# Transposing the activation tiles on the Vector engine instead of TensorE, with transfers that put the blocks in place

## What is computed

```
for t in range(S):                       # per batch and head
    m_new = max(f[t] + m, i[t])
    C = exp(f[t] + m - m_new) * C + exp(i[t] - m_new) * outer(v[t], k[t])
    n = exp(f[t] + m - m_new) * n + exp(i[t] - m_new) * k[t]
    y[t] = sigmoid(o[t]) * (C @ q[t]) / max(|n . q[t]|, 1)
x1 = y as 3072 x 320
x2 = square(relu(x1 @ w_in)) @ w_out
out = elu(x2 @ w2_in) @ w2_out
```

## Time and profile before

| | |
|---|---|
| median of three executions | 845.18 us (845.06 to 847.85) |
| the profiled execution, its own time | 846.34 us |
| its span from first to last instruction | 844.2 us |
| mean granted TensorE clock | 0.982 |
| busy: TensorE, Vector, ScalarE, GpSimd | 834.5, 467.6, 491.7, 264.3 us |

### The profile page before, as it was taken

One profiled execution on the slowest core, in us unless ns is written; L12 is line 12 of the kernel. 1 busy time (PEld: TensorE's weight loads), 2 busy tenths in 40 slices (PEclk: granted clock), 3 DMA queues, 4 the chain that ended last, 5 costly groups with the idle time before them and its releaser, 6 DMA issues.

```text
span 844.2 us, 14970 instructions
## 1 busy us (share of the span) xinstructions
PE 834.5 (99%) x5568; PEld 822.1 (97%) x5568; DVE 467.6 (55%) x823; ACT 491.7 (58%) x1088; POOL 264.3 (31%) x291
## 2 busy tenths in 40 slices
PE   8999999999999999999999999999999999999998
PEld 7899999999999999999999999999999999999998
DVE  5898776665675766656636644444434344444442
ACT  5698676767766767677648754444444444444443
POOL 2654221322222222211102353333334333333332
PEclk7599999999999999999999999999999999999999
DMA  8785444453643443436132300000000000000000
GB/s 252 243 233 147 116 115 108 113 141 90 165 123 105 111 117 108 112 102 159 31 103 76 97 1 2 24 1 24 1 24 1 24 1 24 1 23 3 1 24 24
DMA packets 28257, 66.93 MB, mean 79 GB/s; under 512 B 9401, under 2 KB 15385, under 8 KB 25625
## 3 DMA queue, kind: packets, MB, share of 16 engines
q1 hardware_dynamic: 27608, 64.54, 26.9%
q10 hardware_dynamic: 576, 1.44, 0.5%
HBM read 60.87 MB, written 4.03 MB: 77 GB/s over the span
## 4 chain that ended last, share of the span: by engine, by line
PE 89%; DVE 6%; ACT 2%; issue 1%; DMA 1%; POOL 0%; ACTq 0%; DVEq 0%
PE hps L933 40%; PE acc L947 38%; PE att L858 4%; PE att L823 2%; PE att L849 2%; PE att L863 1%; PE att L838 1%; DVE gate L618 1%; DVE win L690 1%; ACT wts L469 1%; DVE glo L773 1%; DMA wts<-m_rows 1%; PE att L864 1%; DVE win L688 1%; DVE x L673 0%
## 5 line engine op out<-in xcount | busy, mean ns | idle before, releaser
L933 PE MATMUL hps<-xth,win 128*128 128x384 f32 x1280 | 350.6, 339 | 1.0 <-DVE hact L798 1.0
L947 PE MATMUL acc<-wout,ghi 128*128 128x320 f32 x1536 | 347.4, 313 | 0.0
L933 PE MATMUL hps<-xtl,win 128*128 128x384 f32 x768 | 259.9, 338 | 0.0
L947 PEld LDWEIGHTS acc<-wout,ghi 128*128 128x128 f32 x1536 | 257.8, 188 | 0.3 <-POOL glo L431 0.3
L947 PE MATMUL acc<-wout,glo 128*128 128x320 f32 x768 | 237.3, 309 | 0.0
L933 PEld LDWEIGHTS hps<-xth,win 128*128 128x128 f32 x1280 | 229.8, 189 | 1.4 <-issue 1.2
L431 POOL TENSOR_TENSOR glo<-hact,ghi 128x384 fp32r<-128x384 f32 x128 | 130.1, 1016 | 218.6 <-ACT ghi L593 218.5
L773 DVE TENSOR_TENSOR glo<-hact,ghi 128x384 fp32r<-128x384 f32 x128 | 80.1, 626 | 146.5 <-ACT hact L550 145.0
L933 PEld LDWEIGHTS hps<-xtl,win 128*128 128x128 f32 x768 | 145.0, 189 | 0.0
L588 ACT ACTIVATE hact<-hact 128x384 f32<-128x384 f32 x128 | 67.3, 526 | 131.9 <-DVE hact L795 131.9
L947 PEld LDWEIGHTS acc<-wout,glo 128*128 128x128 f32 x768 | 144.1, 188 | 0.0
(11 more groups left out here) (136 smaller groups left out, 665.9 us busy)
## 6 DMA issues: line engine op xcount, KB each, us to landing
raw<-in_qk SPq DMA_DIRECT2D x20, 960.0 KB, 7.2
wts<-m_rows SPq DMA_DIRECT2D x24, 512.0 KB, 8.5
kvo<-in_kvo SPq DMA_DIRECT2D x21, 484.0 KB, 7.9
x<-in_w_all SPq DMA_DIRECT2D x12, 352.0 KB, 7.5
wts<-in_w_all SPq DMA_DIRECT2D x12, 352.0 KB, 2.9
q_of_three<-in_q_trios SPq DMA_DIRECT2D x20, 180.0 KB, 2.6
out_x<-hsum SPq DMA_DIRECT2D x16, 160.0 KB, 1.9
x<-in_w_all ACTq DMA_DIRECT2D x4, 352.0 KB, 6.7
```

Of the source, the lines that this page charges most:

```text
L933: last = nc.tensor.matmul(hps[t % 2][:, 0:NT], win[:, j, w, :], x[:, kk, :], start=(i == 0), stop=(i == len(parts) - 1))
L947: last = nc.tensor.matmul(acc[u][:, 0:DM], g[t % GR][:, cols], wout[:, j, w, :], start=(j == 0 and i == 0), stop=(j == NF - 1 and i == 2))
```

## The change

- **Layer 1, tiles 6 to 23.** At delay 4 the Vector engine transposes the tile by quadrants of 32 partitions: 16 instructions of 32 x 96 elements (`turned`), each of which puts its 32 x 32 blocks on the partitions where they belong, into a new buffer `x1_turned`. `x_hi` and `x_lo` at delay 5 then read that buffer and not PSUM. TensorE's transposes stay for tiles 0 to 5 alone.
- **Layer 2, all 24 tiles.** The Vector engine transposes every 32 x 32 block where it stands (`x2_turned`: two instructions, 320 and 64 elements). Then 16 transfers from SBUF to SBUF on SyncE's queue, 32 partitions and three runs of 128 B each, bring the blocks to their partitions in `x1` (`move_x2`). `x2_hi` and `x2_lo` read from there. The turning stands four steps ahead of its use (`X2_AHEAD`), and `X2_STEPS` is now 5, 9 and 13. A tile is turned only once the transfers of the tile before have landed, as there is one buffer.
- **SyncE's queue** issues the moves between the weight loads of block 7 and the output stores.
- **The last weight slice's** low part on the Vector engine goes from step 0 of block 8 to step 3.
- GpSimd's `copy_rest` goes away, and `m0` lies in another buffer.

```diff
-X2_STEPS = (7, 9, 11)
+X2_STEPS = (5, 9, 13)
+X2_AHEAD = 4
+TURNED = 4
+def turned_at(t):
+    g = tile_at(t, TURNED)
+    return g if g is not None and g >= 2 * T else None
...
+            def move_x2(i):
+                sp.wait_ge(s["x2_turned"], i + 1)
+                wait(sp, "xt_ready", TILES + i - 1)
+                whole = x1[i % 2][:].rearrange("f (k t) -> f k t", t=P)
+                for a in range(4):
+                    for q in range(4):
+                        rows = slice(a * 32, (a + 1) * 32)
+                        sp.dma_start(whole[q * 32:(q + 1) * 32, :, rows], x2_blocks[rows, q::4, :]).then_inc(s["x2_moved"], 16)
...
             wait(sp, "intra_ps", TILES)
-            for n in range(NF, 2 * NF):
-                load_w(sp, n)
+            for n in range(NF, NF + SPARE - 2):
+                load_w(sp, n)
+            for j in range(NF):
+                if j + X2_AHEAD in X2_STEPS:
+                    move_x2(X2_STEPS.index(j + X2_AHEAD))
+                if SPARE - 2 <= j + SPARE - 2 < NF:
+                    load_w(sp, NF + j + SPARE - 2)
+            for block in range(BLOCKS, 2 * BLOCKS):
+                for w in range(T):
+                    if block < 2 * BLOCKS - 1:
+                        move_x2(T * (block + 1 - BLOCKS) + w)
+                    if w == 0 and block > BLOCKS:
+                        for u in range(T):
+                            store(T * (block - 1 - BLOCKS) + u)
...
+            def x2_hi(i, par, u):
+                act.wait_ge(s["x2_moved"], 256 * (i + 1))
+                nc.scalar.activation(xth[par][:, :, u * P:(u + 1) * P], x1[i % 2][:].rearrange("d (k t) -> d k t", t=P), ACT.Copy)\
+                    .then_inc(s["xth_ready"], 1)
...
+            def turned(src, dst, a):
+                rows = src[a * 32:(a + 1) * 32, :].rearrange("t (b f) -> t b f", f=32)
+                blocks = dst.rearrange("f (k t) -> f k t", t=P)[:, :, a * 32:(a + 1) * 32]
+                for q in range(4):
+                    n = len(range(q, src.shape[1] // 32, 4))
+                    last = nc.vector.transpose(blocks[q * 32:(q + 1) * 32, 0:n], rows[:, q::4])
+                    if n < 3:
+                        last = nc.vector.transpose(blocks[q * 32:(q + 1) * 32, 2], rows[:, 6 + q])
+                return last
+
+            def x2_turned(i):
+                dve.wait_ge(s["acc_free"], i + 1)
+                wait(dve, "x2_moved", 256 * i)
+                by_block = x2_blocks.rearrange("f b t -> f (b t)")
+                nc.vector.transpose(by_block[:, 0:DM], x2[:, i, :])
+                nc.vector.transpose(by_block[:, DM:3 * P], x2[:, i, 2 * P:DM]).then_inc(s["x2_turned"], 1)
...
# Vector engine, layer 1, in step t
+                        g = turned_at(t)
+                        if g is not None:
+                            dve.wait_ge(s["x_ready"], g + 1)
+                            for a in range(4):
+                                last = turned(x1[g % 2][:], x1_turned[:], a)
+                            last.then_inc(s["xt_ps"], 1)
...
# Vector engine, layer 2, in step t, behind line 798
-                        if block == BLOCKS and j == 0:
+                        if block == BLOCKS and j == LAG:
                             split_lo(2 * NF - 1)
+                        if block < 2 * BLOCKS - 1 and j + X2_AHEAD in X2_STEPS:
+                            x2_turned(T * (block + 1 - BLOCKS) + X2_STEPS.index(j + X2_AHEAD))
                         if block < 2 * BLOCKS - 1 and j in X2_STEPS:
                             w = X2_STEPS.index(j)
-                            x_lo(T * (block + 1) + w, (block + 1) % 2, w, (A0, A1, A2)[w])
+                            x2_lo(T * (block + 1 - BLOCKS) + w, (block + 1) % 2, w)
...
# TensorE
-                    if BLOCKS - 1 <= block < 2 * BLOCKS - 1 and j in X2_STEPS:
-                        w = X2_STEPS.index(j)
-                        x2_transposed(T * (block + 1 - BLOCKS) + w, w)
```

More of the change, by code:

```diff
@@ L106, in mlstm_two_dense_layers @@
         x1 = [sb(f"x1_{i}", [P, 3 * P]) for i in range(2)]
-        x2_rest = [sb(f"x2_rest_{i}", [P, 2, REM]) for i in range(2)]
+        x1_turned = sb("x1_turned", [P, 3 * P])
         ident = sb("ident", [P, P])
@@ L324, in _, with store @@
                     load_state(g)
-            wait(sp, "intra_ps", TILES)
-            for n in range(NF, 2 * NF):
-                load_w(sp, n)
-            for i in range(TILES):
-                u = i % T
+            def move_x2(i):
[6 more added lines that the diff above has]
+                        sp.dma_start(whole[q * 32:(q + 1) * 32, :, rows], x2_blocks[rows, q::4, :]).then_inc(s["x2_moved"], 16)
+            def store(i):
                 row = batch_of(i) * S + chunk_of(i) * P
                 wait(sp, "acc_free", TILES + i + 1)
-                sp.dma_start(out[row:row + P, :], out_stage[u]).then_inc(out_done[u], 16)
+                sp.dma_start(out[row:row + P, :], out_stage[i % T]).then_inc(out_done[i % T], 16)
+            wait(sp, "intra_ps", TILES)
+            for n in range(NF, NF + SPARE - 2):
[12 more added lines that the diff above has]
+                            store(T * (block - 1 - BLOCKS) + u)
+            for u in range(T):
+                store(TILES - T + u)
             for u in range(T):
@@ L599, in _ @@
                             w = X2_STEPS.index(j)
-                            x_hi(T * (block + 1) + w, (block + 1) % 2, w, (A0, A1, A2)[w])
+                            x2_hi(T * (block + 1 - BLOCKS) + w, (block + 1) % 2, w)
             empty_acc(2 * BLOCKS - 1)
@@ L670, in finish @@
                 dve.wait_ge(s["gated_ready"], g + 1)
-                wait(dve, "xt_ps", g - 1)
+                if g - 2 < 2 * T:
+                    wait(dve, "xt_ps", g - 1)
                 x = x1[g % 2]
@@ L835, in state_added @@
                 else:
-                    pe.wait_ge(s["xt_ready"], g)
+                    pe.wait_ge(s["xt_ready"], min(g, 2 * T))
+                    pe.wait_ge(s["state_ready"], g)
                 for h in range(H):
@@ L873, in x1_transposed @@
                     pe.wait_ge(s["state_ready"], to_state(g + 1))
[L874 to L882, removed]
+                x, bank = x1[g % 2], x_bank(g)
+                for kk in range(3):
+                    last = nc.tensor.transpose(bank[:, kk * P:(kk + 1) * P], x[:, kk * P:(kk + 1) * P], ident[:])
+                last.then_inc(s["xt_ps"], 1)
             def keep_warm(products):
@@ L962, in _ @@
                     g = transposed_at(t)
-                    if g is not None:
+                    if g is not None and g < 2 * T:
                         x1_transposed(g)
```

34 lines of the change are left out of this document (15 added, 19 removed).

## The result

| | before | after |
|---|---|---|
| median | 845.76 us (845.06 to 847.85, 4 executions) | 860.89 us (857.29 to 861.84, 4 executions) |
| the profiled execution, its own time | 846.34 us | 861.84 us |
| its span | 844.2 us | 860.3 us |

The ratio is 1.0158, with a 95% interval of 1.0143 to 1.0173: the changed kernel is 1.6% slower. 914 us was forecast, in a range of 829 to 940.

A forecast was written before the change was run, and what follows sets the result against it. TensorE, busy 99%, was taken to bound the kernel. From 846.3 us, -5.6 (layer 1), -1.5 (late split), +59.2 (blocks 8 to 14) and +17 (block 7) gave 915.4, or 914 us against the median; range 829 to 940.

The forecast's parts named there:

- the cheap case: Layer 2's transfers issue like plain loads, 0.45 us start to start, and only TensorE's terms remain: 830.7 us; chance 0.35.
- the likeliest one: Layer 2's transfers issue like the state's, 0.83 us apart; blocks 8 to 14 take 53.0 us: 914 us; chance 0.53.
- TensorE's terms: Transposes leaving TensorE save 5.6 us in layer 1 and 7.4 in layer 2, the late split 1.5: -14.5 us if all else is hidden.
- The late split: Block 8: moving the last weight split to step 3 removes a stall, 46.0 to 44.55 us, giving back 1.5 us.
- Layer 1 on the Vector engine costs nothing: Layer 1 blocks: 48 transposes at 0.28 us bring the Vector engine to 49.9 of 56.5 us, costed at nothing.
- I take 0.83 us, because the shape of the new ones is the state's: SyncE's queue, layer 2: each of a tile's 16 transfers starts 0.83 us after the one before.
- The formula: Blocks 8 to 14: three consecutive cycles of turning, issues, landing and semaphores, 15.1 us each, plus 7.7 us: 53.0 us.
- Block 7: Moves of tiles 1 and 2 wait behind weight loads, about 4 us each: 53 + 8 = 61 us.
- slices that arrive late: Block 7's term, weight slices coming late: the reason its loss was rounded up to +17 us.
- The rival of cheap issue: The cheap case, chance 0.35: decided at 12.0 us per tile cycle, or 0.62 us per transfer.
- The clock: Layer 2: TensorE idles some 3 us three times a block; a halved clock was costed at nothing.
- the 20 us of the upper bound: Layer 2: half clock would cost two first products 1.4 us more each, up to 20 us in all.

The follow-up runs named there:

- layer1_only: Kernel before plus the last weight split in step 3 and layer 1's tiles 6 to 23 turned by quadrants; layer 2 unchanged: 839.0 us, ratio 0.9904.
- late_split: Kernel before with only the last weight slice's low part moved to step 3 of block 8, from step 0: 845.49 us, ratio 0.9975.
- probes: Kernel before with the late split, plus 32 unneeded SBUF to SBUF transfers of eight shapes in block 8's idle queue: 846.14 us.
- block7_quadrants: Changed kernel with block 7's three tiles turned by quadrants on the Vector engine, without moves: 847.75 us, ratio 1.0016.
- block7_quadrants_lead5: Changed kernel with two turned buffers, turning five steps ahead instead of four, and block 7's tiles by quadrants without moves: 832.84 us, ratio 0.9843.
- spaced_five: Changed kernel with X2_STEPS at 4, 9 and 14 instead of 5, 9 and 13: 872.74 us, ratio 1.0302.
- two_buffers_lead5: Changed kernel with a second turned buffer and the turning five steps ahead of the copy instead of four: 844.37 us, ratio 0.9971.

## Why the prediction was right or wrong

**Direction right, size wrong, range held.** The forecast was 914 us and the change gave 860.89. The range held only by its width: it ran from the cheap case to the forecast's upper end, and the result lies between the two cases, outside the 893 to 940 of the likeliest one.

- **TensorE's terms: right.** 18 x 0.31 = 5.6 us for layer 1; blocks 1 to 6 gave 5.5. The late split: 1.5 predicted; layer1_only and late_split show block 8 at 44.55.
- **Layer 1 on the Vector engine costs nothing: right.** 49.9 us busy per block were expected, 47.9 were measured, and the block is TensorE's 56.53.
- **The step that failed: "I take 0.83 us, because the shape of the new ones is the state's".** It measured 0.64 from start to start. I had named 40 partitions as what could set the state's transfers apart, and then put it aside, since both sides in SBUF and the short runs looked like more. The probes show that the partitions were the difference to 0.6. The formula itself holds: 3 x (0.7 + 15 x 0.64 + 0.05 + 1.9) + 7.7 = 44.5 us per block, and block 11 took 44.57, with one long issue of 0.91 us in it. Blocks 9 and 12 had one of 1.50 and one of 1.27; with what these are over 0.6 added, the formula gives 45.4 and 45.1, and 45.28 and 45.18 were measured. So each block was 8.5 us too long in the sum, 68 us over eight of them.
- **Block 7: the same term.** 53 + 8 was said; with 0.64 it is 44.5 + 8 = 52.5, and 53.24 was measured. The 8 us for moves behind loads are right (3.4 and 3.6 us late), and block7_quadrants takes them away. The "slices that arrive late" show in block 8: at 489.60 the split of a slice is on the chain.
- **The rival of cheap issue** had its point of decision at 0.62 us, and the change landed at 0.64, all but on it. Hence the 44.6 to 45.5 us of blocks 9 and 11 to 13, close to the 44.55 of before, with the 0.93 us of freed TensorE time lost in the wait.
- **The clock: costed at nothing, wrong.** Block 8's stall of 1.0 us showed no loss, but said nothing of gaps over 2 us. About 5 us were lost behind three of them; the 20 us of the upper bound held it.
- **Long issues: not foreseen.** Ten of the 384 took 0.9 to 1.7 us, 7.0 us over 0.6 each when summed, and with one buffer and no slack each lengthens the block it is in.

With the measured issue time the prediction's own sum would have been 915.4 - 68.4 = 847.0 us. The remaining 14.8 us to 861.84 are, by these readings, about 5 us of clock, 7 of long issues, and some 3 of late weight slices and small shifts in blocks 7 and 8; the parts are read from the trace and were not tried one by one. block7_quadrants_lead5 shows them together: it still has the long issues, but a lead that takes most of them up and, in layer 2, no gap over 0.75 us. At 832.84 us it is within 0.4 us of the 832.5 that come out if all but TensorE's terms vanish (846.97 of the same round, less 14.5).

## What to carry to other kernels

Before work is moved to transfers, count the issues: 16 small ones held a queue for 9.6 us here, and a tile was home after 12.2 us, which must be less than the lead from producing it to its first waiting user. Take the price of an issue from a transfer with the same number of partitions and the same memories on both sides, and where a decision hangs on 0.02 us of it, measure it alone. Work added to an engine that takes turns with another belongs into the wait between the two: the same bands gave 875.2 us at the end of a step and 835.6 inside it.

## What the hardware showed that I had not expected

- The partitions of an SBUF to SBUF transfer set its issue time on SyncE's queue: about 0.6 us with 32, 0.72 to 0.79 with 40, 0.64 with 128, with little from the runs.
- An issue now and then takes 0.9 to 2.3 us. The DMA view of the stretch 544.0 to 546.1 us, with the issue of 1.50 us, has a transfer on the queue of instructions (queue, kind: packets, MB, share):

```profile
q1 hardware_dynamic: 274, 0.03, 11.1%
q8 instruction: 1, 0.02, 3.6%
```

  All ten issues over 0.9 us in this kernel, and all twelve in block7_quadrants_lead5, stand beside such a transfer of 16 KB on q8, whose start lies between 0.4 us before and 0.1 us behind that of the issue. That fetching instructions holds the queue is what this suggests; no run changed the fetching.
- TensorE's next product ran at full clock after each gap of 0.6 to 1.2 us in the changed kernel, and of up to 1.8 us in spaced_five; after 2.36, 3.45 and 4.22 us it ran at half. The border is not sharp: in spaced_five a gap of 2.37 us was followed by a product of 2.73 us at a granted clock of 0.50, and one of 2.33 by one of 1.61 at 1.00. In two_buffers_lead5 the clock fell only after TensorE had resumed: the product behind a gap of 3.86 us took 1.87 us, at a mean of 0.79.
- A transpose of the Vector engine that writes other partitions than it reads costs no more than one that stays on its own: of the 288 of 32 x 96, the 72 that stay took 268 ns in the mean, the 216 others 270. But it covers 32 partitions only, where one of 128 x 320 took 510.
